# Moving copies from ScalarE to VectorE, a later h_lo, slot lists in one instruction, and a loop for ScalarE, in a kernel of attention and experts

## Chip, cores and metric

One Trainium2 chip, one core. The metric is the device time of one execution in microseconds (us).

## The reference

```python
for t in range(S):                       # attention with gates, B, H, S, D = 4, 8, 768, 40
    m_new = np.maximum(f_gate[:, :, t] + m, i_gate[:, :, t])
    C = f_stab * C + i_stab * outer(v_t, k_t);  n = f_stab * n + i_stab * k_t
    y[:, :, t] = sigmoid(o_gate[:, :, t]) * (C @ q_t) / np.maximum(np.abs(n @ q_t), 1.0)

logits = x @ w_gate                      # x: 3072 tokens of 320, 8 experts of 384 tokens each
for idx in np.argsort(-logits.flatten()):
    tok, e = idx // E, idx % E           # the next best pair, if the token is free
    if assigned[tok] < 0 and counts[e] < cap: assigned[tok] = e; counts[e] += 1
for e in range(E):
    out[mask_e] = np.maximum(x[mask_e] @ w1[e], 0.0) @ w2[e]      # 320 -> 1024 -> 320

a = x @ w_a; b = x @ w_b                 # 320 -> 1536
return (a * b) @ w_out                   # -> 320
```

All is f32. Each f32 matrix product of the experts is made of three products of a high and a low part (hi x hi, lo x hi, hi x lo), both of type fp32r.

## The kernel before, in words

The kernel has two stages. `attention` writes the tokens to a scratch tensor `xs` and keeps the logits; it ends near 161 us, and nothing of it changes. `experts` does the rest in eight turns, k = 0 to 7, one for each expert, in the order in which the experts become full. While turn k multiplies, a search finds the tokens of the next expert, p = k + 1. Turns 0 to 5 have `beside == "search"`, turn 6 has `"rest"` (the last expert takes what is left, so no search), turn 7 has `None`. The first search runs alone, ahead of turn 0. PE runs turn 0, then a hardware loop over turns 1 to 5, then turns 6 and 7 (`turns`, L807). ScalarE (ACT) and VectorE (DVE) have all eight turns written out (L1141, L1452).

Each engine's work is one list in program order, and semaphores tie the lists together. A turn on each engine:

- PE (L1011): for f = 0 to 7 `up(k, f + 1)` (w1, 8 matmuls into `psA`) and `down(k, f)` (w2, 9 matmuls into `acc[0..2]`), with the search's `count` after the first third of `down`. `up(k, f)` waits for h_lo of f - 2 and `down(k, f)` for h_lo of f (`h_ready`). Then for g = 0 to 11 `pair(k, g + 1)` (w_a into `psA`, w_b into `psB`) and `project(k, g)` (w_out, 9 matmuls into `acc`). Small steps lie between: `slots` at g = 6, `turn_tile(k + 1, 0)` after project of g = 8, `turn_tile(k + 1, 1)` and `(k + 1, 2)` ahead of project of g = 9 and 10. At g = 11 comes `up(k + 1, 0)` ahead of `project(k, 11)`. So at the seam between turns PE runs up(k+1, 0), project(k, 11), up(k+1, 1), down(k+1, 0).
- ACT (L1096): h_hi for each f (L1104), x2_hi (L1113), then per g: a_sb (L1127), ab_hi (L1120), at some g the high parts of the next expert's weights (`high_parts`, L1059). After h_hi of f = 0 of turn k comes `copy_out(k - 1)` (L1079): three copies of `acc[t]` to `o_sb`, which GpSimd scatters to the output (L874), and which `down(k, 0)` waits for (`o_copied`) before it writes `acc`. At g = 8 comes `widen` (L1086): it waits for each of the three gathers of the next tokens and copies the last 64 of 320 columns behind them. `turn_tile` waits for it (`xg_wide`). `columns` (L1054) takes the transposed tokens out of PSUM as x1_hi.
- DVE (L1365): h_lo for each f, the steps of the search (`tally`, `is_full`, `narrow` with its `compare`, L1155), x2_lo, then per g `product`: ab (L1375) and ab_lo (L1379). At g = 5 to 6 `one_hot` (L1287) writes the lists `at_slot` (four of six tiles each), at g = 6 `rows` makes the gather's index, at g = 6, 7, 9 and 10 `low_parts` splits weights (L1310; its last instruction is L1320), at g = 9 and 10 `low` makes x1_lo (L1331). At g = 11 comes h_lo of f = 0 of the next turn (L1431), then `keys` (L1180), seven small steps and the first `compare` of the next search, which `count` waits for.
- GpSimd gathers the tokens with three indirect DMAs (L852) as soon as the index is there, and scatters `o_sb` (L874). SyncE loads weights.

`Count.step` (used on DVE by `keys` and others) lets an instruction signal and has the next one wait for it.

Of the kernel before, what the change touches and what calls it, by code (L numbers as in the profile page):

```python
# [7 lines left out]
ALU = mybir.AluOpType  # L8
# [8 lines left out]
P = 128  # L17
B, H, S, D = 4, 8, 768, 40
E = 8
DM = H * D  # L20
NT = B * S
CAP = NT // E
# [18 lines left out]
def at_least(eng, sem, value):  # L41

    if not isinstance(value, int) or value > 0:
        eng.wait_ge(sem, value)
# [620 lines left out]
ST = TILES // SC  # L665
# [8 lines left out]
def experts(nc, ctx, logit, identf, second, w_a, w_b, w_out, w1, w2, xs, out, fixed):  # L674
# [18 lines left out]
    T = CAP // P  # L693
    FT = F1 // P
# [357 lines left out]
    @block.scalar  # L1052
    def _(act):
        def columns(k, t, ps=psT):  # L1054
            act.wait_ge(sm["t_done"], T * k + t + 1)
            act.copy(x1_hi[:, :, t * P:(t + 1) * P], ps[:, 0:3 * P].rearrange("p (j n) -> p j n", j=3)
                     ).then_inc(sm["x1_hi_ready"], 1)

        def high_parts(k, q):  # L1059
            n = q % 2  # L1060
            act.wait_ge(raw_in[n], 64 * (2 * k + q // 2 + 1))
            if not (isinstance(k, int) and k == 0):
                act.wait_ge(sm["x2_mm"], 3 * k)
            act.copy(w1_hi[q][:, :, :], w1_raw[n][:, :, :]).then_inc(sm["w_hi_done"], 1)
            act.copy(w2_hi[q][:, :, 0:DM], w2_raw[n][:, :, :]).then_inc(sm["w_hi_done"], 1)
            act.copy(w2_hi[q][:, :, DM:], w2_raw[n][:, :, DM - 64:]).then_inc(sm["w_hi_done"], 1)

        def high_out(q):
            act.wait_ge(wo_in[q % 2], 16 * (q // 2 + 1))
            if q == 0:  # L1070
                act.wait_ge(sm["wab_lo"], 2 + 2 * Q)
            act.copy(wo_hi[:, q * GQ:(q + 1) * GQ, :], wo_raw[q % 2]).then_inc(sm["wo_hi_done"], 1)

        for i in range(2):
            act.wait_ge(sm[wab_in[i]], 48)
            act.copy(second[i][:, 0:3, :], wab_raw[:, i, :, :]).then_inc(sm["wab_hi"], 1)
        high_parts(0, 0)

        def copy_out(k):  # L1079
            for t in range(T):  # L1080
                act.wait_ge(sm["out_mm"], T * k + t + 1)

                at_least(act, sm["scattered"], 16 * T * k)
                act.copy(o_sb[:, t, :], acc[t][:, 0:DM]).then_inc(sm["o_copied"], 1)  # L1084

        def widen(k, t):  # L1086
            act.wait_ge(gathered[t], 16 * (k + 1))
            act.copy(xg[:, t, DM:], xg[:, t, DM - 64:DM]).then_inc(sm["xg_wide"], 1)

        for t in range(T):  # L1090
            widen(0, t)
            if t:
                columns(0, t - 1, acc[t - 1])
        columns(0, T - 1, acc[T - 1])

        def turn(k, beside):  # L1096
            early = isinstance(k, int) and k == 0
            for f in range(FT):
                act.wait_ge(sm["up_done"], k * FT + f + 1)

                at_least(act, sm["down_done"], k * (FT - 1) + f - 1)
                if f == 0:
                    at_least(act, sm["x2_mm"], 3 * k)
                act.activation(h_hi[f % 2][:, :], psA[f % 2][:, 0:CAP], ACT.Relu).then_inc(sm["h_hi_ready"], 1)  # L1104
                if f == 0 and not early:
                    copy_out(k - 1)
                if early and f in SPLIT_EARLY:
                    high_parts(0, SPLIT_EARLY[f])
                if early and f == WO_EARLY:
                    high_out(0)  # L1110
            for m in range(3):
                act.wait_ge(sm["x2_mm"], 3 * k + m + 1)
                act.copy(x2_hi[:, m, :], acc[m][:, 0:CAP]).then_inc(sm["x2_hi_ready"], 1)  # L1113

            def ab_high(g):
                act.wait_ge(sm["ab_done"], k * GT + g + 1)
                at_least(act, sm["out_done"], k * (GT - 1) + g - 1)
                if g < 2:
                    at_least(act, sm["out_mm"], T * k)
                act.copy(ab_hi[g % 2][:, :], ab[g % 2][:, :]).then_inc(sm["ab_hi_ready"], 1)  # L1120

            for g in range(GT):
                act.wait_ge(sm["ab_mm"], k * GT + g + 1)
                at_least(act, sm["ab_done"], k * GT + g - 1)
                if early and g == 0:
                    act.wait_ge(sm["wab_lo"], 2 + 2 * Q)
                act.copy(a_sb[g % 2][:, :], psA[g % 2][:, 0:CAP]).then_inc(sm["a_copied"], 1)  # L1127

                if beside and g > 9:
                    columns(k + 1, g - 9)  # L1130
                ab_high(g)
                if early and g < Q - 1:
                    high_out(g + 1)
                if beside and g in SPLIT_AT:
                    high_parts(k + 1, SPLIT_AT[g])
                if beside and g == 8:
                    for t in range(T):
                        widen(k + 1, t)
                if beside and g == 9:
                    columns(k + 1, 0)  # L1140
        for k in range(E):  # L1141
            turn(k, "search" if k < E - 2 else "rest" if k == E - 2 else None)
        copy_out(E - 1)

    @block.vector
    def _(dve):
# [140 lines left out]
        def one_hot(p, i):  # L1287

            if not (isinstance(p, int) and p == 0):

                dve.wait_ge(sm["slots_mm"], p * SC)
            for j in range(ST):
                last = dve.tensor_scalar(at_slot[i][:, j, :], slot[:, :], prow[:, i * ST + j:i * ST + j + 1], None, ALU.is_equal)  # L1293
            last.then_inc(sm["slots_ready"], 1)

        def rows(p):

# [25 lines left out]
        def low_out(q):  # L1323
            dve.wait_ge(sm["wo_hi_done"], q + 1)
            dve.tensor_tensor(wo_lo[:, q * GQ:(q + 1) * GQ, :], wo_raw[q % 2], f32(wo_hi[:, q * GQ:(q + 1) * GQ, :]), ALU.subtract
                              ).then_inc(sm["wo_split"], 1)

        def low(k, t, ps=psT):
            dve.wait_ge(sm["x1_hi_ready"], T * k + t + 1)
            c = slice(t * P, (t + 1) * P)  # L1330
            dve.tensor_tensor(x1_lo[:, :, c], ps[:, 0:3 * P].rearrange("p (j n) -> p j n", j=3), f32(x1_hi[:, :, c]),  # L1331
                              ALU.subtract).then_inc(sm["x1_ready"], 1)
# [15 lines left out]
        low_parts(0, 0)  # L1348
        leave_out()
        propose()  # L1350
        for t in range(T):
            low(0, t, acc[t])
        propose_rest()
# [1 line left out]
        per = ct.n - start + ROUNDS  # L1355
        start -= ROUNDS

        def h_low(k, f):
            dve.wait_ge(sm["h_hi_ready"], k * FT + f + 1)
            dve.scalar_tensor_tensor(out=h_lo[f % 2][:, :], in0=psA[f % 2][:, 0:CAP], scalar=0.0,  # L1360
                                     in1=f32(h_hi[f % 2][:, :]), op0=ALU.max, op1=ALU.subtract).then_inc(sm["h_ready"], 1)

        h_low(0, 0)

        def turn(k, beside):  # L1365

            p = k + 1
            early = isinstance(k, int) and k == 0
            ct.turn(start + p * per)

            def product(g, turned=None):

# [7 lines left out]
                                  ).then_inc(sm["ab_ready"], 1)  # L1380

            search = beside == "search"
            for f in range(FT - 1):
                if search and f:
                    narrow(p, f - 1)
                if search:
                    tally(p, f)
                h_low(k, f + 1)
                if search:
                    is_full(p, f)  # L1390
                if early and f in SPLIT_EARLY:
                    low_parts(0, SPLIT_EARLY[f])
                if early and f == WO_EARLY:
                    low_out(0)
# [10 lines left out]
            for g in range(GT):  # L1405
# [5 lines left out]
                    give()  # L1411
                if beside and g in (5, 6):
                    one_hot(p, 0 if g == 5 else SC - 1)
                if beside and g == 9:
                    low(k + 1, 0)
                if g < GT - 1:
# [2 lines left out]
                if beside == "search":  # L1419
                    if FT + g < ROUNDS:  # L1420
                        narrow(p, FT + g)
                    if g == 3:
                        filled(p)
                    if g == 7:
                        leave_out()
                    if g == 8:
                        propose()
                    if g == 9:
                        propose_rest()
                    if g == GT - 1:  # L1430
                        h_low(k + 1, 0)  # L1431
                        keys()
                if beside == "rest" and g == 3:
                    the_rest(p)
# [8 lines left out]
                    low_out(g + 1)  # L1443
                if beside and g in SPLIT_AT:
                    low_parts(k + 1, SPLIT_AT[g])
            if beside == "rest":
                h_low(k + 1, 0)
            if beside is None:

                dve.wait_ge(sm["scattered"], 16 * T * (E - 1))  # L1450
                dve.tensor_copy(idx_s[:, :], idx_g[:, :]).then_inc(sm["idx_s_ready"], 1)
        for k in range(E):  # L1452
            turn(k, "search" if k < E - 2 else "rest" if k == E - 2 else None)

# [37 lines left out]
```

## Time and profile before

| | us |
|---|---|
| runs of the kernel | 929.12, 937.06, 936.66 |
| their median | 936.66 |
| the profiled execution | 929.12 |
| its span | 927.4 |
| granted clock of TensorE, mean over the span | 0.948 |

The span runs from the first to the last instruction of the profiled execution; its own time is 1.7 us longer. Rows of a timeline give the start in us from the span's start, the length in us, engine, line, operation, output<-inputs, shapes and count, and in brackets how long the engine was idle before, with what ended it. PE is TensorE's matmul queue, PEld its weight loads. The granted clock is 1.00 at 2.4 GHz and 0.50 at 1.2 GHz.

### The profile page before, as it was taken

How to read it: one execution, taken by the hardware profiler on the slowest of the kernel's cores; microseconds unless marked ns; L12 is line 12 of the kernel's file. 1: busy time of each engine (PE TensorE's matmuls, PEld its weight loads, DVE VectorE, ACT ScalarE, POOL GpSimd, SP SyncE). 2: the span in 40 equal slices, each digit the busy share in tenths (PEclk: the TensorE clock that was granted, in tenths of full speed). 3: DMA queues.
4: the chain of work that ended last, by engine and by line, in shares of the span. 5: the costliest groups of instructions: out<-in, count | busy, mean ns of one | idle time of the engine just before them, and what ended most of it. 6: DMA issues, size and time to landing. Idle time of an engine off the chain costs nothing.

```text
span 927.4 us, 16639 instructions
## 1 busy us (share of the span) xinstructions
PE 811.5 (88%) x5858; PEld 754.2 (81%) x5858; DVE 612.4 (66%) x1756; ACT 287.4 (31%) x538; POOL 168.8 (18%) x195
## 2 busy tenths in 40 slices
PE   1999999214699899989998999999899989999995
PEld 0999998213589888988898899889888989989995
DVE  7788898677657766785677657766766683364221
ACT  4444441302233422341234124312522342243221
POOL 6666565171000110010011001100110011011001
PEclk9999999555989999999999999999999999999998
DMA  4866661603202200220032004101300120050000
GB/s 113 251 212 207 212 200 37 204 0 115 74 22 84 85 22 1 63 84 21 0 100 68 0 0 132 35 1 44 102 21 0 63 83 22 1 146 23 1 1 21
DMA packets 51624, 66.63 MB, mean 72 GB/s; under 512 B 6376, under 2 KB 42232, under 8 KB 51576
## 3 DMA queue, kind: packets, MB, share of 16 engines
q1 hardware_dynamic: 37352, 50.31, 17.6%
q0 software_dynamic: 2368, 7.88, 3.0%
q10 hardware_dynamic: 11856, 7.87, 2.8%
q8 instruction: 22, 0.36, 0.2%
q14 instruction: 26, 0.21, 0.1%
HBM read 57.88 MB, written 8.16 MB: 71 GB/s over the span
## 4 chain that ended last, share of the span: by engine, by line
PE 50%; DVE 18%; ACT 4%; DMA 4%; issue 3%; POOL 2%; DVEq 0%; ACTq 0%; POOLq 0%
PE psA L897 20%; PE acc L920 11%; PE psB L897 9%; PE acc L947 7%; DMA xg<-xs_dram,idx_g 4%; DVE at_slot L1293 3%; DVE cmp L1155 2%; DVE ab L1375 2%; POOL xg L852 2%; ACT ab_hi L1120 2%; DVE ab_lo L1379 1%; PE psT L978 1%; PE psT L959 1%; ACT a_sb L1127 1%; PE psT L967 1%
## 5 line engine op out<-in xcount | busy, mean ns | idle before, releaser
L897 PE MATMUL psA<-x_hi,wa 128*128 128x384 f32 x480 | 138.5, 354 | 0.5 <-DVE x_lo L1400 0.4
L897 PE MATMUL psB<-x_hi,wb 128*128 128x384 f32 x480 | 132.0, 339 | 0.0
L852 POOL DMA_INDIRECT xg<-xs_dram,idx_g x24 | 25.1, 1045 | 462.2 <-DVE idx_g L1307 457.3
L1127 ACT COPY a_sb<-psA 128x384 f32<-128x384 f32 x96 | 46.0, 479 | 180.7 <-PE psB L897 180.7
L897 PE MATMUL psA<-x_lo,wa 128*128 128x384 f32 x288 | 98.0, 340 | 0.0
L897 PE MATMUL psB<-x_lo,wb 128*128 128x384 f32 x288 | 96.5, 335 | 0.0
L1375 DVE TENSOR_TENSOR ab<-a_sb,psB 128x384 f32<-128x384 f32 x96 | 53.0, 552 | 64.9 <-ACT a_sb L1127 64.0
L947 PE MATMUL acc<-wo_hi,ab_hi 128*128 128x320 f32 x288 | 93.1, 323 | 1.0 <-DVE ab_lo L1379 1.0
L947 PE MATMUL acc<-wo_hi,ab_lo 128*128 128x320 f32 x288 | 90.0, 313 | 0.0
L947 PE MATMUL acc<-wo_lo,ab_hi 128*128 128x320 f32 x288 | 90.0, 312 | 0.0
L897 PEld LDWEIGHTS psA<-x_hi,wa 128*128 128x128 f32 x480 | 85.3, 193 | 4.1 <-DVE x_lo L1400 2.1
L897 PEld LDWEIGHTS psB<-x_hi,wb 128*128 128x128 f32 x480 | 86.3, 189 | 0.1
L1379 DVE TENSOR_TENSOR ab_lo<-ab,ab_hi 128x384 fp32r<-128x384 f32 x96 | 53.5, 558 | 48.3 <-ACT ab_hi L1120 44.0
L1104 ACT ACTIVATE h_hi<-psA 128x384 fp32r<-128x384 f32 x64 | 31.4, 491 | 173.8 <-PE psA L897 168.8
L897 PE MATMUL psA<-x_hi,w_hi 128*128 128x384 f32 x192 | 74.1, 386 | 10.3 <-DVE w_lo L1320 7.5
L920 PE MATMUL acc<-h_hi,w_hi 128*128 128x384 f32 x192 | 69.8, 363 | 0.0
L1120 ACT CAST ab_hi<-ab 128x384 fp32r<-128x384 f32 x96 | 49.3, 513 | 66.1 <-DVE ab L1375 66.1
L897 PE MATMUL psA<-x_lo,w_hi 128*128 128x384 f32 x192 | 66.0, 344 | 0.0
L920 PE MATMUL acc<-h_lo,w_hi 128*128 128x384 f32 x192 | 65.1, 339 | 0.0
L920 PE MATMUL acc<-h_hi,w_lo 128*128 128x384 f32 x192 | 65.0, 338 | 0.0
L874 POOL DMA_INDIRECT out_dram<-o_sb,idx_s x24 | 23.6, 983 | 206.7 <-ACT o_sb L1084 201.9
L947 PEld LDWEIGHTS acc<-wo_hi,ab_hi 128*128 128x128 f32 x288 | 54.8, 190 | 2.1 <-DVE ab_lo L1379 1.2
(236 smaller groups left out, 1741.9 us busy)
## 6 DMA issues: line engine op xcount, KB each, us to landing
w_raw<-in_w_dram SPq DMA_DIRECT2D x32, 320.0 KB, 3.2
w_raw<-in_w_dram SPq DMA_DIRECT2D x32, 256.0 KB, 3.0
toks<-in_tok_dram SPq DMA_DIRECT2D x24, 324.0 KB, 3.5
qks<-in_qk_dram SPq DMA_DIRECT2D x48, 160.0 KB
w_raw<-in_w_dram SPq DMA_DIRECT2D x64, 64.0 KB, 2.8
gate<-in_tok_dram SPq DMA_DIRECT2D x6, 640.0 KB, 5.9
xs_dram<-y ACTq DMA_DIRECT2D x24, 160.0 KB, 3.3
qst<-in_qk_dram ACTq DMA_DIRECT2D x48, 60.0 KB
```

The lines of the kernel that those rows point to most:

```text
L852: pool.indirect_dma_start(out=xg[:, t, 0:DM], out_offset=None, in_=xrows, in_offset=bass.IndirectOffsetOnAxis(ap=idx_g[:, t:t + 1], axis=0 ...
L874: pool.indirect_dma_start(out=out, out_offset=bass.IndirectOffsetOnAxis(ap=idx_s[:, t:t + 1], axis=0), in_=o_sb[:, t, :], in_offset=None). ...
L897: last = pe.matmul(ps, w, x, start=(n == 0), stop=(n == len(steps) - 1))
L920: last = pe.matmul(acc[m][:, 0:CAP], w[q][:, f % FQ, c], x[n][:, :], start=(f == 0 and j == 0), stop=(f == FT - 1 and j == 2))
L947: last = pe.matmul(acc[t][:, 0:DM], x[n][:, c], w[:, g, :], start=(g == 0 and j == 0), stop=(g == GT - 1 and j == 2))
L1104: act.activation(h_hi[f % 2][:, :], psA[f % 2][:, 0:CAP], ACT.Relu).then_inc(sm["h_hi_ready"], 1)
L1120: act.copy(ab_hi[g % 2][:, :], ab[g % 2][:, :]).then_inc(sm["ab_hi_ready"], 1)
L1127: act.copy(a_sb[g % 2][:, :], psA[g % 2][:, 0:CAP]).then_inc(sm["a_copied"], 1)
L1155: dve.scalar_tensor_tensor(out=cmp[:, :, :], in0=key[lv][:, :].unsqueeze(2).broadcast_to([P, TILES, 16]), scalar=start_at[:, lv:lv + 1] if ...
L1293: last = dve.tensor_scalar(at_slot[i][:, j, :], slot[:, :], prow[:, i * ST + j:i * ST + j + 1], None, ALU.is_equal)
L1375: dve.tensor_tensor(ab[g % 2][:, :], a_sb[g % 2][:, :], psB[g % 2][:, 0:CAP], ALU.mult).then_inc(sm["ab_done"], 1)
L1379: dve.tensor_tensor(ab_lo[g % 2][:, :], ab[g % 2][:, :], f32(ab_hi[g % 2][:, :]), ALU.subtract).then_inc(sm["ab_ready"], 1)
```

## The change

Five edits, all in `experts`:

1. ACT's turns run through `turns`, as PE's do: turn 0, a loop over turns 1 to 5, turns 6 and 7.
2. `copy_out` leaves ACT. DVE copies `acc` to `o_sb` at the end of its turn k.
3. h_lo of f = 0 of turn k + 1, on DVE, was issued at the end of turn k ahead of `keys`; it now is the first step of turn k + 1, behind `keys` and behind the three copies.
4. `widen` leaves ACT. DVE runs it at g = 8 ahead of `product(9)`, and for k = 0 after `propose`. On ACT `columns` for k = 0 stand without it.
5. `one_hot` makes its six tiles with one `tensor_tensor` over 768 columns instead of six `tensor_scalar` over 128.

```diff
@@ scalar
-        def copy_out(k):
-            for t in range(T):
-                act.wait_ge(sm["out_mm"], T * k + t + 1)
-
-                at_least(act, sm["scattered"], 16 * T * k)
-                act.copy(o_sb[:, t, :], acc[t][:, 0:DM]).then_inc(sm["o_copied"], 1)
-
-        def widen(k, t):
-            act.wait_ge(gathered[t], 16 * (k + 1))
-            act.copy(xg[:, t, DM:], xg[:, t, DM - 64:DM]).then_inc(sm["xg_wide"], 1)
-
         for t in range(T):
-            widen(0, t)
-            if t:
-                columns(0, t - 1, acc[t - 1])
-        columns(0, T - 1, acc[T - 1])
+            columns(0, t, acc[t])
...
-                if f == 0 and not early:
-                    copy_out(k - 1)
...
-                if beside and g == 8:
-                    for t in range(T):
-                        widen(k + 1, t)
...
-        for k in range(E):
-            turn(k, "search" if k < E - 2 else "rest" if k == E - 2 else None)
-        copy_out(E - 1)
+        turns(act, turn)
@@ vector
-            for j in range(ST):
-                last = dve.tensor_scalar(at_slot[i][:, j, :], slot[:, :], prow[:, i * ST + j:i * ST + j + 1], None, ALU.is_equal)
-            last.then_inc(sm["slots_ready"], 1)
+            dve.tensor_tensor(at_slot[i][:, :, :], prow[:, i * ST:(i + 1) * ST].unsqueeze(2).broadcast_to([P, ST, P]),
+                              slot[:, :].unsqueeze(1).broadcast_to([P, ST, P]), ALU.is_equal).then_inc(sm["slots_ready"], 1)
...
+        def widen(k):
+            for t in range(T):
+                dve.wait_ge(gathered[t], 16 * (k + 1))
+                dve.tensor_copy(xg[:, t, DM:], xg[:, t, DM - 64:DM]).then_inc(sm["xg_wide"], 1)
...
         propose()
+        widen(0)
         for t in range(T):
             low(0, t, acc[t])
...
-        h_low(0, 0)
-
         def turn(k, beside):
...
+            h_low(0)
             for f in range(FT - 1):
...
-                h_low(k, f + 1)
+                h_low(f + 1)
...
+                if beside and g == 8:
+                    widen(k + 1)
...
                     if g == GT - 1:
-                        h_low(k + 1, 0)
                         keys()
...
-            if beside == "rest":
-                h_low(k + 1, 0)
             if beside is None:
 
                 dve.wait_ge(sm["scattered"], 16 * T * (E - 1))
                 dve.tensor_copy(idx_s[:, :], idx_g[:, :]).then_inc(sm["idx_s_ready"], 1)
+            for t in range(T):
+                dve.wait_ge(sm["out_mm"], T * k + t + 1)
+
+                at_least(dve, sm["scattered"], 16 * T * k)
+                dve.tensor_copy(o_sb[:, t, :], acc[t][:, 0:DM]).then_inc(sm["o_copied"], 1)
```

## Rows read from the trace of the kernel before

**Rows 1.** The page: busy time, share of the span, instructions of TensorE.

```profile
PE 811.5 (88%) x5858; PEld 754.2 (81%) x5858; DVE 612.4 (66%) x1756; ACT 287.4 (31%) x538; POOL 168.8 (18%) x195
```

**Rows 2.** The page: the chain that ended last, shares of the span by engine.

```profile
PE 50%; DVE 18%; ACT 4%; DMA 4%; issue 3%; POOL 2%; DVEq 0%; ACTq 0%; POOLq 0%
```

**Rows 3.** Timeline 406 to 424 us, PE, DVE, ACT: start, length, engine, line, [idle before].

```profile
412.46 0.44 PE L897 MATMUL psA<-x_hi,w_hi 128*128 128x384 f32 x1 [0.82 <-DVE x_lo L1331]
...
414.15 0.49 ACT L1104 ACTIVATE h_hi<-psA 128x384 fp32r<-128x384 f32 x1 [1.67 <-PE psA L897]
...
414.58 1.31 ACT L1084 COPY o_sb<-acc 128x320 f32<-128x320 f32 x3
...
415.01 0.29 DVE L1320 TENSOR_TENSOR w_lo<-w_raw,w_hi 128x128 fp32r<-128x128 f32 x1
...
415.23 0.55 DVE L1360 SCALAR_TENSOR_TENSOR h_lo<-psA,h_hi 128x384 fp32r<-128x384 f32 x1
...
416.65 0.34 PE L920 MATMUL acc<-h_hi,w_hi 128*128 128x384 f32 x1
...
417.28 0.62 DVE L1155 SCALAR_TENSOR_TENSOR cmp<-key,start_at,steps_of 128x384 bf16<-128x384 f32 x1
...
417.96 0.26 PE L959 MATMUL psT<-ohc,cmp 128*128 128x64 bf16 x3 [0.62 <-DVE cmp L1155]
```

**Rows 4.** Timeline 418 to 437 us, PE: the same pair of steps one f later.

```profile
421.02 0.34 PE L920 MATMUL acc<-h_hi,w_hi 128*128 128x384 f32 x1
...
421.54 0.26 PE L959 MATMUL psT<-ohc,cmp 128*128 128x64 bf16 x3
```

**Rows 5.** Groups of instructions, shapes apart: busy us, mean ns, on DVE.

```profile
L1317 DVE TENSOR_TENSOR w_lo<-w_raw,w_hi 128x640 fp32r<-128x640 f32 x32 | 26.4, 826 | 1.0
...
L598 DVE TENSOR_TENSOR num<-num,psO 128x328 f32<-128x328 f32 x24 | 11.9, 496 | 10.8 <-PE psO L461 10.7
...
L1178 DVE TENSOR_TENSOR ohc<-prop,givenc 128x192 bf16<-128x192 f32 x7 | 2.5, 359 | 0.2
```

**Rows 6.** Timeline 205 to 240 us, DVE and ACT: the first slot lists and the third widening copy.

```profile
209.96 3.99 DVE L1293 TENSOR_SCALAR at_slot<-slot,prow 128x128 bf16<-128x128 bf16 x24
...
222.93 0.24 ACT L1088 COPY xg<-xg 128x64 f32<-128x64 f32 x1 [1.34 <-DMA xg<-xs_dram,idx_g]
```

**Rows 7.** Timeline 398 to 406 us, PE, DVE, ACT.

```profile
399.81 0.49 PE L886 MATMUL psT<-identf,xg 128*128 128x128 f32 x3
...
400.77 0.29 DVE L1320 TENSOR_TENSOR w_lo<-w_raw,w_hi 128x128 fp32r<-128x128 f32 x1
...
400.86 0.24 ACT L1088 COPY xg<-xg 128x64 f32<-128x64 f32 x1 [1.89 <-DMA xg<-xs_dram,idx_g]
401.01 0.47 ACT L1127 COPY a_sb<-psA 128x384 f32<-128x384 f32 x1
...
401.52 0.56 DVE L1375 TENSOR_TENSOR ab<-a_sb,psB 128x384 f32<-128x384 f32 x1 [0.46 <-ACT a_sb L1127]
...
405.37 0.52 PE L886 MATMUL psT<-identf,xg 128*128 128x128 f32 x3 [2.26 <-DVE x_lo L1331]
```

**Rows 8.** The chain, its longest pieces: start us, us, what.

```profile
317.99 1.88 PE acc L947 x9
319.87 2.38 PE psA L897 x8
...
483.51 4.86 DMA xg<-xs_dram,idx_g
...
835.89 1.32 PE acc L947 x9
837.22 1.39 PE psA L897 x8
```

**Rows 9.** Windows: PE, PEld, DVE, ACT, POOL busy (instructions), granted clock, DMA share, GB/s.

```profile
405.00:409.00 4.00, 3.63 (x24) 3.67 (x25) 3.11 (x9) 2.45 (x5) 0.00 (x0) 1.00 0.17 63
493.00:497.00 4.00, 4.00 (x18) 4.00 (x19) 2.75 (x8) 2.45 (x5) 0.00 (x0) 0.63 0.00 2
```

More of the change, by code:

```diff
@@ L1356, in _ @@
         start -= ROUNDS
[L1358 to L1361, printed above, removed]
-        h_low(0, 0)
         def turn(k, beside):
@@ L1369, in turn, with h_low @@
             ct.turn(start + p * per)
+            def h_low(f):
+                dve.wait_ge(sm["h_hi_ready"], k * FT + f + 1)
+                dve.scalar_tensor_tensor(out=h_lo[f % 2][:, :], in0=psA[f % 2][:, 0:CAP], scalar=0.0,
+                                         in1=f32(h_hi[f % 2][:, :]), op0=ALU.max, op1=ALU.subtract).then_inc(sm["h_ready"], 1)
             def product(g, turned=None):
```

## Prediction

> **What bounds the kernel now.** I read the page first: TensorE is busy for 88% of the span, VectorE for 66% and ScalarE for 31% [rows 1]. The chain that ended last agrees: half of it is PE and 18% DVE; ACT and DMA have 4% each [rows 2]. So a microsecond costs only where PE then stands still, and those places have to be looked up in the timeline. In each of the eight turns there are two places that the change touches. One is the seam between two turns: PE goes from up(k+1, 0) over project(k, 11) and up(k+1, 1) into down(k+1, 0) without a wait and then waits 0.62 us for the first cmp of the next search [rows 3]. The other is g = 8 and 9, where PE transposes the gathered tokens: it waits 2.26 us there in turn 1, for x_lo of the tile before [rows 7].
>
> **The change part by part, at the seam.** Now DVE ends the weight split at 415.30 (415.01 + 0.29), starts h_lo for f = 0 at 415.23 and the keys after it, and starts cmp at 417.28 [rows 3]. Instructions on DVE start some 0.07 us before the end of the one ahead (415.23 against 415.30). So h_lo takes 0.48 us of the queue, and the seven key steps the other 1.57. Changed, the keys come first: cmp starts at 415.23 + 1.57 = 416.80 and frees DVE at 416.80 + 0.62 - 0.07 = 417.35. Then come the three copies of acc. A DVE pass over 128x328 from PSUM takes 0.496 us [rows 5], so 320 columns take 0.49 and 0.42 of the queue; ACT's three take 1.31 in all [rows 3]. They end their share at 418.61; their wait for project(k, 11) is long over, since ACT ran the same copies from 414.58. Queued behind them is h_lo of f = 0, 418.61 to 419.16, and PE waits for it before down(k+1, 0). With the 0.06 us that PE took after cmp (417.90 to 417.96), down starts at 419.22 where it started at 416.65 [rows 3]: 2.57 us late. The wait for cmp is now covered: down to count is 0.52 us where nothing is late [rows 4], so count comes at 419.74 for 417.96. **+1.78 us at each of the five seams with a search behind them.** The seam into turn 6 runs the keys too but has no count that used to wait: +2.57. The seam into turn 7 has no keys: 415.23 + 3 x 0.42 + 0.55 + 0.06 = 417.10 against 416.65, +0.45. Together 5 x 1.78 + 2.57 + 0.45 = **+11.9**. At 0.44 us each, as on ACT (1.31 / 3), or 0.49 with no overlap, a seam costs 0.06 to 0.2 us more; at 0.33, 320 columns at the rate below and no fixed part, 0.27 less: some 1.5 us either way in all. That o_sb is written 3 us later delays only the scatter, which nothing here waits for.
>
> **Transposes and widening.** In turn 1 ACT waits for the third gather, copies at 400.86, and only then serves a_sb at 401.01, so ab(9) starts at 401.52, although DVE had been free since 401.06 (400.77 + 0.29) [rows 7]. With widen on DVE, behind the same weight split, ACT's a_sb is ready early and DVE runs three copies of 64 columns first. The trace has no such copy; below each lies the 0.166 us pace of at_slot (3.99 / 24, 128 columns [rows 6]) and above the 0.29 us of w_lo on 128 columns [rows 7]. I take 0.2, near the first, since 64 columns is the smaller form: ab(9) at 401.66, alone +0.1. PE however gets xg_wide of tile 0 at about 401.3 instead of before 399.81: it stands 1.5 us there, and pair(10) behind it (399.81 + 0.25 + 3.04 = 403.1 now) ends at 404.6. The next transposes start at 405.37, for x_lo, whatever PE does before: the 2.26 us gap is split into 1.5 and 0.8 us and the total stays. Cost zero as long as x_lo stays the later one; were PE itself the bound there, 1.5. Before turn 0 the first copy waits for DVE's proposals, but the third one ends it, at 222.93 [rows 6], when DVE is free: zero.
>
> **The slot lists.** Six compares of 128 columns become one of 768. Two f32-fed instructions give the rate: 359 ns for 192 columns and 826 for 640 [rows 5], 1.04 ns a column, so 768 take 0.96 us, 0.89 of the queue, against 6 x 0.166 = 1.00 [rows 6]. Upper bound: cmp, with the same kind of broadcast, takes 0.62 for 384 [rows 3], which extends to 1.06. Lower bound: twice the rate would give 0.56. I take 0.96, as 640 columns is the nearest row. That saves 0.4 us of DVE per turn ahead of ab(7), the index and the gather. Where the gather is late (4.86 us in turn 2 [rows 8]) all of it counts, and a_sb no longer queues behind the ACT copy (0.5 us); where DVE is late, part goes to the widening copies. I take -0.2 and -0.5 in turn, mean -0.35, times seven: **-2.5**. The first search has this on the open path: **-0.35**. The last o_copied is 0.06 us later on DVE: **+0.1**.
>
> **The clock.** After a stall of this length PE sometimes runs at 1.2 GHz for a while. The window at 493 has a granted clock of 0.63 and that at 405 has 1.00 [rows 9], after gaps of the same place; of ten gaps of 2.1 to 3.0 us in this trace (three near 232 to 254 us, seven at the transposes) five were followed by such a stretch. One costs 1.88 - 1.32 plus 2.38 - 1.39 = 1.55 us [rows 8]. At the transposes 0.82 us of it is covered, since PE waits that long for x_lo just after [rows 3], leaving about 0.75. The split gaps (1.5 and 0.8 us) should not trigger it: four of the five stretches go, -3.0. The new gap at six seams (2.57 us) should trigger it in four, at full price since the f loop has no slack: +6.2. Together **+3.2**, with 0 and +9.3 less or more as bounds for the new ones (none or all six) and 0 to -3.0 for the old.
>
> **Loop on ACT.** The turns of ACT become a loop; PE already runs one. Its last step before the seam and its h_hi at 414.15 lie 1.67 us apart [rows 3], and h_lo, which needs h_hi, is 3.4 us later than now: a loop turn is hidden up to 5 us. Register waits on PE show nothing: down to count takes 0.52 us in a looped turn [rows 4]. Cost zero.
>
> One page speaks against the loop. The Trainium skill, Runtime: NRT & Kernel Launch, section Instruction fetch mechanics, says that a taken branch out of the fetched pages stalls the engine until a DMA has brought the target. No row here shows such a stall on PE's loop, and it would change the sum only beyond the 5 us of cover; that is the fourth rival.
>
> **Sum.** 11.9 - 2.5 - 0.35 + 0.1 + 3.2 = +12.4 us. The profiled execution took 929.12 us (span 927.4 and 1.7 around it), which gives 941.5. It is the fastest of three; their median is 936.66. I add the sum to the median: **949.1 us**.
>
> **The rivals.** (1) *The clock goes the good way:* the seams trigger nothing and the old stretches vanish: 12.4 - 6.2 = +6.2, 942.9. For it: gaps of 2.5 us passed without a fall five times in ten. Against it: five did not. (2) *The clock goes the bad way:* all six seams fall and the old ones stay: 12.4 + 3.1 + 3.0 = +18.5, 955.2. For it: the seam gaps are as long as those of now. Against: the split. (3) *The merged compare is fast, and the kernel gets faster:* at 0.56 us and below, each list saves another 0.4 us, 1.6 a turn ahead of the gather, and PE's 2.26 us wait can take all of it: 12.4 - 8 x 1.6 = -0.4, 936.3, and with (1) 930.1. It is on the faster side from 0.57 us down. Against: 359 ns for 192 columns with bf16 out is no faster than f32. (4) *ACT's loop stalls:* a fetch of twice the gather's 4.86 us [rows 8] would stick out by 4.7 us at each of six passages: +28, 977. Against: PE's loop.
>
> **How the numbers follow.** Forecast 0.57 (its own range 943 to 955), rival 1 0.17, rival 2 0.12, rival 3 0.10, rival 4 0.04. Slower by over 1% means above 946.0, faster below 927.3; that is about what a measurement of this kernel tells from none, with runs from 929.12 to 937.06. Slower: 0.75 of the forecast, rival 2 and rival 4, 0.59. Faster: 0.04, out of rival 3. Same: the remaining 0.37. The range leaves out rival 4 and most of rival 3: 938 to 958.
>
> **What would show it.** Right: at each seam DVE runs keys, cmp, three o_sb, h_lo, and PE's down waits about 2.5 us on h_lo; the cmp wait is gone; the transposes of tile 0 wait about 1.5 us on widen, and those of tile 1 under 1; at_slot near 960 ns; stretches at 1.2 GHz behind seams rather than behind transposes. Wrong: a seam wait below 1.5 us, at_slot far from 0.96, or ACT idle by "issue" at its loop ends with PE waiting for h_hi or a_sb.

## The result, and the profile after

| | before | after |
|---|---|---|
| median of 16 runs | 932.37 us | 939.62 us |
| lowest to highest | 929.12 to 937.06 | 936.88 to 943.06 |
| profiled execution, its span | 929.12, 927.4 us | 947.86, 946.1 us |
| granted clock, profiled execution | 0.948 | 0.944 |

The kernel became slower by 0.8%: ratio 1.008, 95% interval 1.006 to 1.010. Forecast were 949.1 us and +12.4; measured are 939.62 and +7.25. The two profiles exaggerate this: that of before is one of its fastest executions and that of after lies above all 16 timed ones. So the traces are read here turn by turn, and the total from the medians.

The page of after has the same picture as [rows 1, 2], with more of the chain on DVE:

```profile
PE 820.5 (87%) x5858; PEld 757.7 (80%) x5858; DVE 619.5 (65%) x1644; ACT 273.4 (29%) x490; POOL 169.3 (18%) x195
...
PE 48%; DVE 23%; issue 5%; ACT 4%; DMA 2%; POOL 1%; ACTq 0%; DVEq 0%; POOLq 0%
```

The waits of after, all turns (total us, times, longest):

```profile
PE acc L920 <- DVE h_lo L1349: 14.5, 7, 2.4
...
PE psT L886 <- DVE xg L1308: 6.2, 6, 1.0
PE psT L886 <- DVE x_lo L1313: 6.2, 7, 1.5
```

The first one is new: seven seams, 2.3 to 2.4 us in each that has keys, 0.2 in the one that has none. The other two stand for the one wait of 2.1 to 3.0 us that PE had for x_lo at the transposes [rows 7]. The timeline of the seam into turn 2, which answers to [rows 3]:

```profile
421.36 0.29 DVE L1297 TENSOR_TENSOR w_lo<-w_raw,w_hi 128x128 fp32r<-128x128 f32 x1
...
421.57 0.17 DVE L1162 TENSOR_SCALAR sign<-best 128x24 int32<-128x24 int32 x1
...
423.07 0.62 DVE L1133 SCALAR_TENSOR_TENSOR cmp<-key,start_at,steps_of 128x384 bf16<-128x384 f32 x1
...
423.61 1.28 DVE L1437 COPY o_sb<-acc 128x320 f32<-128x320 f32 x3
424.80 0.55 DVE L1349 SCALAR_TENSOR_TENSOR h_lo<-psA,h_hi 128x384 fp32r<-128x384 f32 x1
...
425.50 0.45 PE L920 MATMUL acc<-h_hi,w_hi 128*128 128x384 f32 x1 [2.41 <-DVE h_lo L1349]
...
426.13 0.26 PE L959 MATMUL psT<-ohc,cmp 128*128 128x64 bf16 x3
```

That is the order that was forecast: keys, cmp, three copies, h_lo, and PE starts down when h_lo is there. From the end of the weight split to down it is 3.85 us where the forecast had 3.92 (419.22 - 415.30) and the kernel before has 1.35 (416.65 - 415.30), so down starts 2.50 us late. Count no longer waits for cmp.

The transposes of turn 5, which answer to [rows 7]:

```profile
768.77 0.39 DVE L1308 COPY xg<-xg 128x64 f32<-128x64 f32 x3
769.01 0.55 PE L886 MATMUL psT<-identf,xg 128*128 128x128 f32 x3 [1.04 <-DVE xg L1308]
769.08 0.55 DVE L1356 TENSOR_TENSOR ab<-a_sb,psB 128x384 f32<-128x384 f32 x1
769.73 0.51 ACT L1103 CAST ab_hi<-ab 128x384 fp32r<-128x384 f32 x1 [2.55 <-DVE ab L1356]
...
772.99 0.52 PE L886 MATMUL psT<-identf,xg 128*128 128x128 f32 x3 [0.64 <-DVE x_lo L1313]
```

PE stands 1.04 us for widen and 0.64 for x_lo, where 1.5 and 0.8 were forecast. The three copies take 0.39 us together; a_sb is early and ab(9) follows them at once. One thing was not forecast: ab ends at 769.63 and ab_hi starts 0.10 us later; before, 401.52 + 0.56 was followed by ab_hi after 0.03.

Turn 1 shows a cost of widen on VectorE that was not forecast either. VectorE waits for the third gather there, and ab(9) and x_lo wait behind it:

```profile
407.60 0.20 DVE L1308 COPY xg<-xg 128x64 f32<-128x64 f32 x1 [0.68 <-DMA xg<-xs_dram,idx_g]
...
411.62 0.52 PE L886 MATMUL psT<-identf,xg 128*128 128x128 f32 x3 [1.41 <-DVE x_lo L1313]
```

Groups of after, which answer to [rows 5, 6]: the merged list takes 954 ns for 768 columns (forecast 960), a copy of acc 483 (forecast 490).

```profile
L1270 DVE TENSOR_TENSOR at_slot<-prow,slot 128x768 bf16<-128x768 f32 x32 | 29.1, 954 | 0.3
...
L1437 DVE COPY o_sb<-acc 128x320 f32<-128x320 f32 x24 | 10.3, 483 | 0.7 <-PE acc L947 0.7
```

Windows of after, columns as in [rows 9]: behind the seams into turns 2 and 3 (first and last line) PE has a granted clock of 0.50, at the transposes of turn 2 (498.0 to 502.0) 1.00:

```profile
427.00:430.00 3.00, 3.00 (x11) 2.35 (x10) 1.10 (x5) 0.00 (x0) 1.18 (x2) 0.50 0.30 109
498.00:502.00 4.00, 3.33 (x19) 3.03 (x20) 2.82 (x9) 2.93 (x6) 0.00 (x0) 1.00 0.49 141
516.00:522.00 6.00, 6.00 (x21) 5.04 (x22) 1.98 (x7) 0.00 (x0) 2.27 (x3) 0.50 0.22 82
```

To tell clock from waits I take turn lengths: from the first matmul of down(k, 0) to the first of down(k + 1, 0), in the timeline. Stars mark a stretch at 1.2 GHz that begins inside the turn or within 0.5 us of its start.

| turn | 1 | 2 | 3 | 4 | 5 | 6 |
|---|---|---|---|---|---|---|
| before | 87.19 | 88.08* | 87.77* | 88.10* | 87.19 | 78.02 |
| after | 89.62 | 90.39* | 91.67* | 90.43* | 88.78 | 77.57 |

A turn is called undisturbed where it has no such stretch and VectorE does not wait for a gather in it. An undisturbed search turn takes 88.78 us (turn 5) instead of 87.19, +1.59, and a stretch behind a seam adds 1.6 us (a double one, in turn 3, 2.9). Turn 1 of after has no stretch but takes 89.62, 0.84 more than turn 5: 0.75 of that is there once PE has stood at its transposes, behind the late gather shown above.

### The profile page after: what moved, and what is told of

It reads as the page before. It is cut to its first block, busy times and chain, and to the rows that moved or that the text cites. A ratio compares the mean times of both kernels' runs of the same rounds, so it can differ in the third digit from the quotient of the medians.

```text
span 946.1 us, 16640 instructions
## 1 busy us (share of the span) xinstructions
PE 820.5 (87%) x5858; PEld 757.7 (80%) x5858; DVE 619.5 (65%) x1644; ACT 273.4 (29%) x490; POOL 169.3 (18%) x195
## 4 chain that ended last, share of the span: by engine, by line
PE 48%; DVE 23%; issue 5%; ACT 4%; DMA 2%; POOL 1%; ACTq 0%; DVEq 0%; POOLq 0%
PE psA L897 18%; PE acc L920 11%; PE psB L897 8%; PE acc L947 6%; DVE at_slot L1270 2%; DVE ab L1356 2%; DVE w_lo L1294 2%; DMA xg<-xs_dram,idx_g 2%; DVE cmp L1133 2%; ACT ab_hi L1103 2%; DVE w_lo L1290 2%; DVE ab_lo L1360 1%; DVE w_hi L1292 1%; PE psT L978 1%; DVE o_sb L1437 1%
## 5 line engine op out<-in xcount | busy, mean ns | idle before, releaser
L897 PE MATMUL psA<-x_hi,wa 128*128 128x384 f32 x480 | 136.1, 348 | 0.5 <-DVE x_lo L1382 0.4
L897 PE MATMUL psA<-x_hi,w_hi 128*128 128x384 f32 x192 | 76.5, 399 | 13.5 <-DVE w_lo L1297 7.5
L897 PEld LDWEIGHTS psA<-x_hi,wa 128*128 128x128 f32 x480 | 83.1, 188 | 4.1 <-DVE x_lo L1382 2.1
L920 PE MATMUL acc<-h_hi,w_hi 128*128 128x384 f32 x192 | 73.0, 380 | 14.5 <-DVE h_lo L1349 14.5
L897 PE MATMUL psA<-x_lo,w_hi 128*128 128x384 f32 x192 | 67.9, 354 | 0.0
L920 PE MATMUL acc<-h_lo,w_hi 128*128 128x384 f32 x192 | 67.3, 350 | 0.0
L920 PE MATMUL acc<-h_hi,w_lo 128*128 128x384 f32 x192 | 67.2, 350 | 0.0
```

What stands on the lines that cost most here:

```text
L897: last = pe.matmul(ps, w, x, start=(n == 0), stop=(n == len(steps) - 1))
L920: last = pe.matmul(acc[m][:, 0:CAP], w[q][:, f % FQ, c], x[n][:, :], start=(f == 0 and j == 0), stop=(f == FT - 1 and j == 2))
```

## The experiments

Ten kernels beside the changed one, each timed against the kernel before on the same chip. "Turn" is the length of an undisturbed search turn. The ratio is not the quotient of the two medians, and the two can differ by 1 to 2 us: for before_lists the medians give -4.35 us and the ratio -6.5, for before_widen -6.9 and -5.9. slots_split and widen_act have four runs, before_lists and before_widen five, the others ten or more.

| kernel | median us | before, same chip | ratio, interval | turn |
|---|---|---|---|---|
| after | 939.62 | 932.37 | 1.008 (1.006 to 1.010) | 88.78 |
| act_unrolled | 938.81 | 931.85 | 1.0066 (1.0043 to 1.009) | 88.3 |
| slots_split | 945.69 | 931.85 | 1.0161 (1.009 to 1.0231) | 89.16 |
| widen_act | 947.35 | 931.85 | 1.0147 (1.0105 to 1.0189) | none undisturbed |
| copies_act_h_first | 923.78 | 931.85 | 0.991 (0.9882 to 0.9938) | 86.50 |
| before_loop | 936.63 | 933.01 | 1.0038 (1.001 to 1.0067) | none undisturbed |
| copies_act | 928.88 | 933.01 | 0.9952 (0.9924 to 0.9979) | 87.12 |
| h_first | 933.78 | 933.01 | 1.0005 (0.9979 to 1.003) | 88.0 |
| h_copies_keys | 933.51 | 933.01 | 1.0007 (0.9982 to 1.0031) | 88.23 |
| before_lists | 930.36 | 934.71 | 0.993 (0.9894 to 0.9966) | 86.76 |
| before_widen | 927.79 | 934.71 | 0.9937 (0.9907 to 0.9968) | 86.9 to 87.0 |

**act_unrolled: the loop on ACT.**

```diff
-        turns(act, turn)
+        for k in range(E):
+            turn(k, "search" if k < E - 2 else "rest" if k == E - 2 else None)
```

> The changed kernel with ACT's eight turns written out again. Theory (all of the loss comes from VectorE's queue at the seams and the clock): the loop is free; undisturbed search turns stay at 88.8 us as in the changed kernel, the median stays +7 us from before (+5 to +9). Rival (the loop on ACT costs, by branches or register waits): turns fall by 0.3 us or more, the median by 2 us or more.

Turns 2, 3 and 5 took 88.30, 88.30 and 88.28 us, 0.49 less than 88.78: of the turns the rival holds, the loop costs half a microsecond a turn. Where it comes from stands in the timeline of turn 5 at the place shown above for after:

```profile
762.26 0.44 DVE L1309 COPY xg<-xg 128x64 f32<-128x64 f32 x3
762.50 0.55 PE L886 MATMUL psT<-identf,xg 128*128 128x128 f32 x3 [0.85 <-DVE xg L1309]
762.61 0.55 DVE L1357 TENSOR_TENSOR ab<-a_sb,psB 128x384 f32<-128x384 f32 x1
763.19 0.51 ACT L1103 CAST ab_hi<-ab 128x384 fp32r<-128x384 f32 x1 [2.34 <-DVE ab L1357]
```

ab ends at 763.16 and ab_hi starts 0.03 us later; in the loop it was 0.10. Over all of g this is so in every looped turn of after (0.11 us in most) and in none of turns 0, 6 and 7, which are written out there too (0.03). The delays reach PE at two places: laid beside act_unrolled, turn 5 of after is some 0.2 us late from the first project on, and 0.38 at the transposes of tile 0; 0.49 at the end. The medians moved less than this says: by the ratios (1.008 and 1.0066) it is 1.3 us, where 5 x 0.49 would be 2.4; the intervals overlap, so the medians alone would not have shown it, and the 2 us that the rival put on the median are not borne out. At the loop's ends h_hi of f = 0 starts 0.20 us after PE's last matmul, where it is 0.04 with written-out turns. ACT has stood idle for 1.8 us there, so a stall shorter than that would not show; a longer one did not occur.

**slots_split: the merged lists.**

```diff
-            dve.tensor_tensor(at_slot[i][:, :, :], prow[:, i * ST:(i + 1) * ST].unsqueeze(2).broadcast_to([P, ST, P]),
-                              slot[:, :].unsqueeze(1).broadcast_to([P, ST, P]), ALU.is_equal).then_inc(sm["slots_ready"], 1)
+            for j in range(ST):
+                last = dve.tensor_scalar(at_slot[i][:, j, :], slot[:, :], prow[:, i * ST + j:i * ST + j + 1], None, ALU.is_equal)
+            last.then_inc(sm["slots_ready"], 1)
```

> The changed kernel with six tensor_scalar of 128 columns for each slot list again. Theory: the merged list saves 0.09 us of VectorE's queue per list where DVE is late, so turns get longer by 0.1 to 0.35 us (88.9 to 89.15) and the whole by 1 to 2.5 us over the changed kernel (+8 to +10 from before). Rival (the index and the gather are hidden anyway): turns stay at 88.8 us.

Turns 5 and 4 took 89.16 and 89.35 us, 0.38 and 0.57 more than 88.78: the theory's direction, a little more than its 0.35. The median missed: 13.8 us over before, where +8 to +10 was expected, from four runs (943.03 to 954.85) with a wide interval. A part that the theory lacked is in turn 1, 90.38 us without a stretch: VectorE stands 1.02 us ahead of the third widening copy, for its gather, and PE waits 1.74 us for x_lo.

**widen_act: the widening copies back on ACT.**

```diff
+        def widen(k, t):
+            act.wait_ge(gathered[t], 16 * (k + 1))
+            act.copy(xg[:, t, DM:], xg[:, t, DM - 64:DM]).then_inc(sm["xg_wide"], 1)
...
+                if beside and g == 8:
+                    for t in range(T):
+                        widen(k + 1, t)
...
-                if beside and g == 8:
-                    widen(k + 1)
```

> The changed kernel with the widening copies back on ACT. Theory: PE's wait at the transposes is one gap of 2.1 to 2.6 us again instead of 1.0 and 0.6 us, and stretches at 1.2 GHz come back behind it in some turns; undisturbed turns stay within 0.3 us of 88.8, those with a stretch there are 0.6 to 0.9 us longer, the median is 2 to 4 us over the changed kernel (+9 to +11 from before). Rival (the split of the gap does nothing, widen on VectorE costs DVE time): turns get shorter by 0.2 us or more and the median falls.

PE's wait at the transposes was one gap of 2.0 to 2.5 us again, and stretches at 1.2 GHz came back behind it in turns 0, 1, 3 and 5, beside those behind four of six seams. Windows of this kernel, behind a seam and behind transposes:

```profile
426.00:429.00 3.00, 3.00 (x12) 2.61 (x10) 1.12 (x4) 0.00 (x0) 1.61 (x2) 0.53 0.40 147
412.00:415.00 3.00, 3.00 (x11) 3.00 (x11) 2.80 (x8) 1.38 (x3) 0.00 (x0) 0.50 0.00 0
```

Turns 3 and 5, with a stretch behind the transposes alone, took 90.12 and 90.00 us, 1.2 to 1.3 over 88.78, where 0.6 to 0.9 was expected. The median lies some 6 us over the changed kernel (by the ratios, 1.0147 and 1.008; 8 by the medians, from four runs): the theory's direction, more than its 2 to 4.

**copies_act_h_first: the seam undone.** The same edit puts ACT's turns back as written out.

```diff
-        turns(act, turn)
+        for k in range(E):
+            turn(k, "search" if k < E - 2 else "rest" if k == E - 2 else None)
+        copy_out(E - 1)
...
+                if f == 0 and not early:
+                    copy_out(k - 1)
...
                     if g == GT - 1:
+                        h_low(k + 1, 0)
                         keys()
...
-            for t in range(T):
-                dve.wait_ge(sm["out_mm"], T * k + t + 1)
-
-                at_least(dve, sm["scattered"], 16 * T * k)
-                dve.tensor_copy(o_sb[:, t, :], acc[t][:, 0:DM]).then_inc(sm["o_copied"], 1)
```

> The changed kernel with its seam undone: copies of acc back on ACT (its turns written out), h_lo of f = 0 ahead of the keys; widen and the merged lists stay changed. Theory: no gap ahead of down at the seams, no stretch at 1.2 GHz behind them, undisturbed search turns 87.19 - 0.2 = 87.0 us, and since the gap at the transposes is split as well, no stretches there: the median is 3 to 6 us below before (ratio 0.994 to 0.997). Rival (widen or the merged lists carry part of the loss): turns of 87.3 us or more and a median at or above before.

Turns 2 to 5 took 86.49 to 86.51 us, 1.79 less than act_unrolled's 88.29: that is the price of the seam, forecast as 1.78. The seam is as in [rows 3], with the old wait for cmp:

```profile
415.38 0.55 DVE L1354 SCALAR_TENSOR_TENSOR h_lo<-psA,h_hi 128x384 fp32r<-128x384 f32 x1
415.85 0.17 DVE L1173 TENSOR_SCALAR sign<-best 128x24 int32<-128x24 int32 x1
...
418.12 0.26 PE L959 MATMUL psT<-ohc,cmp 128*128 128x64 bf16 x3 [0.62 <-DVE cmp L1144]
```

No turn from 1 to 6 has a stretch at 1.2 GHz. It differs from the kernel before only by the merged lists and widen on VectorE, and it is faster than both: ratio 0.991. The gain was larger than expected, 0.5 us more in a turn (86.50 for 87.0) and some 8 us in the whole for 3 to 6: the price of the seam was right, what lists and widening give back was taken too low.

**before_loop: ACT's loop alone, in the kernel before.**

```diff
-        for k in range(E):
-            turn(k, "search" if k < E - 2 else "rest" if k == E - 2 else None)
+        turn(0, "search")
+        turn(1, "search")
+        with act.Fori(2, E - 2) as k:
+            turn(k, "search")
+        turn(E - 2, "rest")
+        turn(E - 1, None)
```

> The kernel before with only ACT's loop, over turns 2 to 5 (turns 0 and 1 stay written out, so that every wait is for a number above zero). Theory from the last runs (register waits on ACT start ab_hi 0.11 us after ab instead of 0.03): the looped turns take 0.3 to 0.5 us more than 87.19 where no stretch at 1.2 GHz lies in them, turn 1 does not change, and the median rises by 1 to 2 us. Rival (the 0.49 us per turn of the changed kernel came from an interplay with its late seam): looped turns stay at 87.2 us.

Each looped turn of the profile had a stretch behind the transposes, so the length without one is not seen. With one, turns 2, 3 and 4 took 88.17, 88.69 and 88.83 us, where before has 88.08, 87.77 and 88.10 with one; turn 5 took 88.54 with one. The wait at the transposes was 2.2 to 2.9 us there, against 2.1 to 2.6 in before. Turn 1, written out and expected unchanged, took 89.45 for 87.19: PE waited 3.8 us at its transposes, and a stretch followed. So one profile does not part the loop from chance here. The median rose by 3.6 us (933.01 to 936.63), more than the 1 to 2 expected; the loop costs in the kernel before too, but how much of this is the clock is not shown.

**copies_act, h_first, h_copies_keys: which piece holds the seam.** In copies_act the copies of acc are on ACT and h_lo stays behind the keys. In h_first h_lo is ahead of the keys and the copies stay behind them. In h_copies_keys the order is h_lo, copies, keys.

```diff
@@ copies_act: as in copies_act_h_first, without
+                        h_low(k + 1, 0)
@@ h_first, against the changed kernel
                     if g == GT - 1:
+                        h_low(k + 1, 0)
                         keys()
@@ h_copies_keys, against the changed kernel
                     if g == GT - 1:
+                        h_low(k + 1, 0)
+                        copy_out(k)
                         keys()
```

> The changed kernel with the copies of acc back on ACT (turns written out), h_lo of f = 0 still behind the keys. Theory: VectorE's queue ahead of h_lo holds the keys alone, 1.5 us: down starts 1.2 to 1.3 us late, the seam costs 0.5 to 0.6 us and undisturbed search turns take 86.50 + 0.55 = 87.05 us. Since the gap is short, no stretch at 1.2 GHz behind the seams. Median 2 to 4 us below before. Rival (the order of h_lo and keys alone carries the loss): turns at 88.3 us.

> The changed kernel (looped ACT, copies on VectorE) with h_lo of f = 0 ahead of the keys, the three copies still behind them. Theory: PE now waits at down for the first copy of acc instead of for h_lo: gap 1.6 us, turns 88.78 - 0.8 = 88.0 us. Rival (only h_lo holds PE at the seam): gap under 0.3 us and turns near 87.0 us.

> The changed kernel with the order h_lo, three copies, keys on VectorE (looped ACT). Theory: down starts on time, but the first count waits for cmp, which comes 1.3 us later than in the kernel before: PE waits about 2.0 us there instead of 0.62, turns take 87.0 + 1.3 = 88.2 us, and stretches at 1.2 GHz can follow this gap too. Rival (the copies cost nothing where h_lo is not behind them): turns near 87.0 us.

In their turns all three came out by the theory: 87.12 (87.05 expected), 88.0 (88.0) and 88.23 us (88.2). Turn 1 is longer in copies_act (87.94) and in h_first (88.26). PE's wait at the seam, in this order, is for h_lo, for the first copy, for cmp:

```profile
416.88 0.44 PE L920 MATMUL acc<-h_hi,w_hi 128*128 128x384 f32 x1 [1.15 <-DVE h_lo L1360]
```

```profile
420.38 0.44 PE L920 MATMUL acc<-h_hi,w_hi 128*128 128x384 f32 x1 [1.53 <-DVE o_sb L1441]
```

```profile
420.40 0.26 PE L959 MATMUL psT<-ohc,cmp 128*128 128x64 bf16 x3 [1.85 <-DVE cmp L1133]
```

So the seam is not lost through h_lo alone: VectorE's queue there holds three things that PE wants within 2 us, and with the copies in it one of them is always late. Of the 1.79 us the order of h_lo and keys holds 0.62 (87.12 - 86.50) and the copies in the queue the other 1.17 (88.29 - 87.12). Between h_first and the changed kernel the medians, as ratios, differ by 7 us. Some 5.5 of these are the turns, 0.8 us in each search turn and 0.6 in turn 6; the rest may be the clock, since h_first's gaps of 1.5 us were followed by no stretch at 1.2 GHz.

**before_lists and before_widen: the two halves that gain, alone.** The edits are the `one_hot` and the `widen` hunks of the change, put into the kernel before.

```diff
@@ before_widen
-                if beside and g == 8:
-                    for t in range(T):
-                        widen(k + 1, t)
@@ on VectorE
+                if beside and g == 8:
+                    widen(k + 1)
                 if beside and g == 9:
                     low(k + 1, 0)
```

> The kernel before with only the merged slot lists. Theory: undisturbed search turns get shorter by 0.35 to 0.4 us (86.8), the gap at the transposes stays one of 2.1 to 2.6 us, and stretches at 1.2 GHz stay behind it; the median falls by 2 to 3.5 us. Rival (merged lists gain only together with widen on VectorE): turns 87.1 to 87.2 us.

> The kernel before with only the widening copies on VectorE. Theory: the gap at the transposes is split into 1.1 to 1.4 and about 1 us, no stretch at 1.2 GHz follows it, undisturbed turns are 0.3 us shorter (86.9), and the median falls by 4 to 6 us, most of it by the clock. Rival (the split gap does not matter to the clock): stretches behind the transposes as in the kernel before, median down by 2 us at most.

Merged lists: turns of 86.73 and 86.79 us, 0.43 less, and three stretches behind the transposes as before; median -4.35 us (2 to 3.5 expected). The gap at the transposes got shorter too, 1.7 to 2.1 us with one of 3.0. Widen on VectorE: turns of 86.91 to 87.02, only 0.17 to 0.28 less, but no stretch in turns 1 to 7, and the median falls by 6.9 us (5.9 by the ratio, 3.0 to 8.7 by its interval; 4 to 6 expected). 0.23 us in six search turns and 0.57 in turn 6 make 2 of these; what is left, 4 to 5 us with a wide margin, goes to the clock, whose median in the timed runs rose from 0.945 to 0.953. PE stands there for 1.25 and 0.55 to 0.63 us instead of once for 2.3.

**Gaps and the clock over all profiles.** For each of PE's gaps at these two places, and for the three waits for weight splits in turn 0, I counted whether a stretch at 1.2 GHz began in it or behind it:

| gap | length us | followed |
|---|---|---|
| seams of after, act_unrolled, slots_split, widen_act | 2.2 to 2.4 | 10 of 24 |
| count of h_copies_keys | 1.8 to 1.9 | 2 of 5 |
| seams of h_first | 1.5 to 1.6 | 0 of 6 |
| seams of copies_act | 1.1 to 1.2 | 0 of 6 |
| transposes, one gap (before, widen_act, before_loop, before_lists) | 1.7 to 3.8 | 18 of 28 |
| transposes, split (eight kernels, turns 0 to 5) | 0.8 to 1.4, then 0.5 to 1.7 | 0 of 48 |
| transposes of turn 6 in the same eight kernels, one gap | 1.2 to 1.8 | 0 of 8 |
| waits for weight splits in turn 0, twelve kernels | 2.5 | 26 of 36 |

The shortest gap with a stretch behind it is 1.82 us. The 20 undivided gaps of 1.1 to 1.8 us in the third, fourth and seventh row had none, so these runs do not tell whether it is the division that helps or the length of the longest piece. Of the last row, 1 of 3 is in the profile of before and 3 of 3 in that of after; turn 0 took 99.3 us in the one and 104.7 in the other, of which the seam explains 2.5.

## Why the prediction was wrong

The direction was right and 939.62 lies in the range, but the predicted time was 9.5 us too high. 4.3 us of that is the base, and 5.0 the term of the clock: forecast +3.2, about -1.8 left by the measurement. Two more steps failed, and that they cancel is luck: the lists and the widening gave 2.75 us more than forecast, and the loop, put at zero, cost 2.45. Term by term:

- **The seam, +11.9.** Right. Forecast 1.78 us a turn, measured 1.79. The seam into turn 7, forecast +0.45, cost 77.49 - 76.91 = 0.58 (act_unrolled against copies_act_h_first). With 2.57 left as it was for the seam into turn 6 (the seam into turn 2 shows 2.50) that is 5 x 1.79 + 2.57 + 0.58 = 12.1.
- **The lists and the widening, -2.5.** Mis-sized by half. The list's duration was right (954 against 960 ns), and the lists alone gave 0.43 us a search turn and 0.66 in turn 6, 3.2 in all (before_lists). What failed is the step "the total stays. Cost zero" for the widening. The three copies take 0.39 us instead of 0.6, and PE's wait at the transposes is split into 1.04 and 0.64 us, 1.7 in all for 2.3; alone that gave 2.0 us (before_widen). Both together shorten a search turn by 87.19 - 86.50 = 0.69 instead of 0.35, turn 6 by 1.11: 6 x 0.69 + 1.11 = 5.25, with turn 0 taken as the others.
- **Before turn 0, -0.35.** Right for the lists: four in 3.57 us against 3.99. The +0.1 for the last o_copied was not measured apart.
- **The loop, zero.** Wrong: 5 x 0.49 = +2.45. "Register waits on PE show nothing" was no evidence for ACT. The place looked at on PE, down to count, had nothing late in it; the place on ACT where the loop costs is one where ACT stands idle and waits for DVE, and it then starts 0.08 us later than with written-out turns. Rival 4 described another cost, a stall at the ends of the loop. The Trainium skill, Runtime: NRT & Kernel Launch, section Instruction fetch mechanics, has such a stall for a taken branch out of the fetched pages; no stall longer than the 1.8 us for which ACT is idle there was seen, so rival 4 did not come about. ACT's two idle stretches ended by "issue", 5.0 and 2.9 us in turns 6 and 7, are in act_unrolled too.
- **The clock, +3.2.** Wrong in sign. Without it the terms measured add up to 12.1 - 5.25 + 2.45 - 0.35 + 0.1 = +9.05, close to the 9.15 forecast because the errors of lists, widening and loop cancel. The medians differ by 7.25, so about -1.8 is left for the clock, 5 us from the forecast. That is a remainder and was not measured by itself: the interval of the ratio (5.6 to 9.3 us) makes it -3.5 to +0.3, and turn 1's extra 0.84 us, which the sum leaves out, would make it lower. The granted clock of the timed runs agrees with the sign, since its median is 0.946 for before and 0.953 for after. The mechanism was as put: seams do trigger stretches, each costs 1.5 to 1.6 us (1.55 forecast), and the split gap triggers none. Two sizes failed. Of the new gaps 10 in 24 were followed, not 4 in 6, which makes +4.0 instead of +6.2. And I counted what the split gives back in one profile, 0.75 us each for four; before_widen puts it at some 4 to 5 us. The profiled execution of before was the fastest of the sixteen, so it probably showed fewer stretches than most. About 1 us of the clock's share stays without a source.
- **The base.** The sum was added to the median of three runs, 936.66 us. Sixteen runs have 932.37. That is 4.3 us of the 9.5; the ratio forecast, 1.013, missed 1.008 by less.

Rival 1, the clock going the good way (+6.2), came nearest in size, but its mechanism was half right: old stretches gone, new ones there, fewer. Rival 3 fell with 954 ns.

## What to carry to other kernels

Where an engine hands over several results within a couple of microseconds, its queue there is the resource: work out the start of each from the sum of what is ahead of it, as that held here to 0.1 us, and keep copies that another idle engine can do out of it. A wait of TensorE that cannot be removed was cheaper in two pieces with matmuls between than in one: at these places the clock fell only behind undivided ones of 1.8 us and more. A copy that waits for a DMA holds up all that its engine has queued behind it, so put it where the DMA has landed. Gains and losses by the clock are to be taken from many runs, not from one profile, and a base of three runs is too thin for a forecast of one per cent.

## What the runs showed that was not expected

- An operation on ACT that waits for DVE started 0.03 us after it with written-out turns and 0.10 to 0.11 us after it in the loop, 0.49 us per turn on PE in all.
- After gaps of 2.2 to 2.4 us of PE at the seams a stretch at 1.2 GHz followed in 10 of 24 cases, after seams of 1.6 us or less and after split gaps in none of 60.
- Moved to VectorE, the third widening copy waited 0.68 us for its gather in turn 1 of after and 1.02 us in that of slots_split, and held up ab(9) and x_lo.
- Three f32 copies of 64 columns in SBUF took 0.39 us of VectorE together, although one lasts 189 ns.

What stays open: why slots_split and before_loop lost more in the median than their undisturbed turns show (13.8 and 3.6 us), what in the loop delays ACT, and how much of the clock's share lies in turn 0, where every kernel has stretches of its own behind the weight splits. None of these was tried.
